# Token mixing with its result transposed, and channel mixing that reads it so

## The reference

```python
theta = x @ w_theta
zr, zi = x * np.cos(theta), x * np.sin(theta)
y = einsum('ts,bsd->btd', w_tok_r, zr) + einsum('ts,bsd->btd', w_tok_i, zi)
u = x + y
m = u + np.maximum(u @ w_ch, 0.0)
gate_pre = sum(conv_w[k] * shifted_by(m, 4 - k) for k in range(5))   # along the tokens
out = (sigmoid(gate_pre) * (m @ w_val)) @ w_out
```

## Time and profile before

| what | value |
|---|---|
| time, median of 3 runs | 741.42 us (741.24 to 741.75) |
| time of the profiled execution | 742.81 us |
| its span (first to last instruction) | 741.0 us |
| PE busy | 688.6 us |
| DVE / ACT / POOL busy | 404.3 / 293.2 / 219.9 us |
| instructions on PE | 3936 matmuls, 3936 weight loads |
| mean granted TensorE clock | 0.97 of full |

### The profile page before, as it was taken

The page is one execution under the profiler, slowest core; times in us unless marked ns, Lnnn a source line. Parts: engine busy times, 40 slices in busy tenths (PEclk is TensorE's granted clock), DMA queues, the critical chain, the costliest instruction groups (busy, mean ns, idle before and its releaser), DMA issues. The chain is left out here.

```text
span 741.0 us, 13752 instructions
## 1 busy us (share of the span) xinstructions
PE 688.6 (93%) x3936; PEld 595.8 (80%) x3936; DVE 404.3 (55%) x973; ACT 293.2 (40%) x752; POOL 219.9 (30%) x267
## 2 busy tenths in 40 slices
PE   4999999999847999999999999987499999999997
PEld 3888888888736888888888888867399999999995
DVE  2666666766517345554564455640936745654770
ACT  3666656666414232231332313313344344435332
POOL 3313223131102221221212212303752463355222
PEclk9999999999969999999999999996889999999999
DMA  5445546464230000600150032064102102200111
GB/s 172 148 139 179 169 149 200 136 189 152 69 119 29 29 15 0 226 19 9 44 182 28 0 140 102 13 206 151 43 1 86 50 35 85 85 24 19 44 43 43
DMA packets 43072, 66.27 MB, mean 89 GB/s; under 512 B 3744, under 2 KB 20384, under 8 KB 42912
## 3 DMA queue, kind: packets, MB, share of 16 engines
q1 hardware_dynamic: 43040, 65.89, 27.4%
HBM read 47.00 MB, written 18.87 MB: 89 GB/s over the span
## 5 line engine op out<-in xcount | busy, mean ns | idle before, releaser
L809 POOL TENSOR_TENSOR z_lo<-z_raw,z_hi 128x512 fp32r<-128x512 f32 x48 | 61.4, 1300 | 213.0 <-ACT z_hi L843 213.0
L245 ACT ACTIVATE probs<-masked,neg_max 128x260 f32<-128x260 f32 (+1 forms) x192 | 92.4, 482 | 69.4 <-DVE neg_max L290 69.2
L972 PE MATMUL acc<-z_hi,w2h 128*128 128x512 f32 x288 | 114.3, 397 | 0.0
L972 PE MATMUL acc<-z_lo,w2h 128*128 128x512 f32 x288 | 112.3, 390 | 0.0
L972 PE MATMUL acc<-z_hi,w2l 128*128 128x512 f32 x288 | 112.3, 390 | 0.0
L290 DVE CUSTOM_DVE_ANT_0 masked<-ps_s,mask 128x260 f32<-128x260 f32 (+1 forms) x192 | 69.0, 403 | 57.7 <-PE ps_s L361 53.7
L1249 DVE SCALAR_TENSOR_TENSOR taps<-m_raw,conv_w,taps 128x384 f32<-128x384 f32 x128 | 76.2, 666 | 0.0
L875 DVE TENSOR_TENSOR xT_lo<-ps_x,xT_hi 128x512 fp32r<-128x512 f32 x24 | 16.6, 690 | 98.3 <-ACT xT_hi L830 98.3
L401 PE MATMUL ps_o<-v_sb,probsT 128*128 128x64 f32 x384 | 66.5, 268 | 0.0
L361 PE MATMUL ps_s<-k_sb,q_sb 64*128 64x260 f32 (+1 forms) x384 | 53.4, 398 | 11.0 <-POOL mask L199 11.0
L972 PEld LDWEIGHTS acc<-z_hi,w2l 128*128 128x128 f32 x288 | 54.1, 188 | 11.7
(11 more groups left out here) (91 smaller groups left out, 1472.9 us busy)
## 6 DMA issues: line engine op xcount, KB each, us to landing
k_sb<-kT SPq DMA_DIRECT2D x16, 396.0 KB, 4.8
q_sb<-qT SPq DMA_DIRECT2D x16, 384.0 KB, 4.3
v_sb<-vP SPq DMA_DIRECT2D x16, 384.0 KB
x_scratch<-x_sb SPq DMA_DIRECT2D x16, 384.0 KB, 3.6
x_nat<-x_scratch SPq DMA_DIRECT2D x24, 256.0 KB, 3.3
x_res<-x_scratch SPq DMA_DIRECT2D x24, 256.0 KB, 4.2
u_scratch<-u_sb SPq DMA_DIRECT2D x24, 256.0 KB, 2.9
u_nat<-u_scratch SPq DMA_DIRECT2D x8, 768.0 KB, 4.6
```

Of the source, the lines that this page charges most:

```text
L245: nc.scalar.activation(probs[e][:, i, lo:hi], masked[2 * t + e][:, lo:hi], ACT.Exp, bias=neg_max[:, s, e, i:i + 1], scale=-1.0, accum_out= ...
L809: nc.gpsimd.tensor_tensor(z_lo[s % ZR][:, part, :], z_raw[:, part, :], z_hi[s % ZR][:, part, :].bitcast(F32), ALU.subtract).then_inc(z_lo_ ...
L972: last = nc.tensor.matmul(acc[t][:], l, r, start=s == 0 and m == 0 and a == 0, stop=s == T - 1 and m == 1 and a == 2)
```

## The change

In block 2, z becomes the stationary operand and the token weights the moving one, so that a bank holds channels by tokens. A result of 512 channels by 768 tokens fills six banks so: bank j < 4 holds channel tile j with tokens 0 to 511 (matmuls of 512 columns), bank 4 holds tokens 512 to 767 of channel tiles 0 and 1, bank 5 those of tiles 2 and 3 (matmuls of 256 columns, two halves in a bank). The residual has to be transposed too: ACT copies `ps_x` once more, to `xT_raw`, SP stores that to a new DRAM tensor `xT_scratch` in rows of 128 tokens, and the residual is loaded from there, bank by bank, once all six tiles of the batch are stored. u is stored transposed (`uT_scratch`).

In block 3, u is loaded as it is needed, so that the 96 transposes, their two banks and ACT's copy to `uT` go. `ps_c` has four banks in place of two. ACT casts `uT` to `uT_hi` (`hi_u`) from SBUF, and does so for chunk n+2 behind the four `hi_m(n+1)`, no longer between those of `hi_g(n)`. In front of the first body it casts chunks 0 and 1, then does `hi_m(0)`. POOL's body is as it was.

```diff
         x_res = [sb(f"x_res{r}", [P, C]) for r in range(RR)]
+        xT_raw = [sb(f"xT_raw{r}", [P, CB, P]) for r in range(XR)]
...
+            def bank_of(scr, b, j):
+
+                if j < CB:
+                    return scr[bass.ds(b, 1), j * P:(j + 1) * P, 0:C].rearrange("o p t -> (o p) t")
+                k = 2 * (j - CB)
+                return scr[bass.ds(b, 1), k * P:(k + 2) * P, C:S].rearrange("o (k p) t -> p (o k) t", p=P)
...
+            def load_res(b, j):
+
+                if j < RR:
+                    for t in range(T):
+                        sp.wait_ge(xT_out[t], 16 * (b + 1))
+                        sp.sem_inc(sp_gate2, 1)
+                sp.wait_ge(u_done, T * (b + 1) + j - RR + 1)
                 sp.sem_inc(sp_gate2, 1)
...
+                sp.dma_start(two_halves(x_res[j % RR], j), bank_of(xT_scr, b, j)).then_inc(res_in[j % RR], 16)
+
+            def store_xT(b, s):
+                sp.wait_ge(xT_raw_done, T * b + s + 1)
+                sp.sem_inc(sp_gate2, 1)
+                sp.dma_start(xT_scr[bass.ds(b, 1), :, s * P:(s + 1) * P].rearrange("o (k p) t -> p (o k) t", p=P),
+                             xT_raw[s % XR][:]).then_inc(xT_out[s], 16)
...
                 act.wait_ge(turned2, n + 1)
+                wait_count(act, xT_out[(s - XR) % T], 16 * (b + 1) if s >= XR else 16 * b)
+                nc.scalar.copy(xT_raw[s % XR][:], ps_x[:]).then_inc(xT_raw_done, 1)
                 wait_count(act, theta_done, n - XR + 1)
                 nc.scalar.copy(xT_hi[s % XR][:], ps_x[:]).then_inc(xT_hi_done, 1)
...
+            def block_of(s, k, bank, cols, first):
+
+                for m in range(2):
+                    at = ((1 - m) * T + s) * S
+                    w = (w2h[:, at + cols.start:at + cols.stop], w2l[:, at + cols.start:at + cols.stop])
+                    z = (z_hi[s % ZR][:, m, k * P:(k + 1) * P], z_lo[s % ZR][:, m, k * P:(k + 1) * P])
+                    for a, (l, r) in enumerate(split_passes(z, w)):
+                        last = nc.tensor.matmul(bank, l, r, start=first and s == 0 and m == 0 and a == 0,
+                                                stop=s == T - 1 and m == 1 and a == 2, skip_group_check=True)
+                return last
...
+                    if j < CB:
+                        last = block_of(s, j, acc[j][:], slice(0, C), True)
+                    else:
+                        for h in range(2):
+                            last = block_of(s, 2 * (j - CB) + h, acc[j][:, h * (S - C):(h + 1) * (S - C)],
+                                            slice(C, S), h == 0)
...
+        ps_c, ps_v, ps_o = banks("ps3_c", CB), banks("ps3_v", 2), banks("ps3_o", 2)
...
-                wait_count(sp, turned, CB * (n - 1))
+                wait_count(sp, m_done, CB * (n - 1))
+                wait_count(sp, uT_lo_done, CB * (n - 1))
                 sp.sem_inc(sp_gate3, 1)
...
+            def hi_u(b, c, k):
                 n = 2 * b + c
...
-                act.wait_ge(turned, CB * n + k + 1)
-                wait_count(act, m_done, CB * (n - 1))
-                nc.scalar.copy(uT[c][:, k, :], ps_t[k % 2][:, 0:L]).then_inc(uT_done, 1)
+                if k == 0:
+                    act.wait_ge(u_in[c], 16 * (b + 1))
+                wait_count(act, mixed, CB * (n - 1))
                 wait_count(act, uT_lo_done, CB * (n - 1))
-                nc.scalar.copy(uT_hi[c][:, k, :], ps_t[k % 2][:, 0:L]).then_inc(uT_hi_done, 1)
+                nc.scalar.copy(uT_hi[c][:, k, :], uT[c][:, k, :]).then_inc(uT_hi_done, 1)
...
                     for k in range(CB):
                         hi_g(b, c, k)
-                        if nxt2:
-                            evac_u(*nxt2, k)
                     if nxt:
                         for k in range(CB):
                             hi_m(*nxt, k)
+                    if nxt2:
+                        for k in range(CB):
+                            hi_u(*nxt2, k)
                     evac_out(b, c)
...
                     for k in range(CB):
                         values(b, c, k)
-                        if nxt2:
-                            turn(*nxt2, k)
```

More of the change, by code:

```diff
@@ L701, in mix_tokens @@
         u_out = [sem(f"u_out{r}") for r in range(RR)]
+        xT_out = [sem(f"xT_out{t}") for t in range(T)]
         w3_in = [sem(f"w3_in{j}") for j in range(4)]
@@ L775, in body @@
                         load_x(b + 1, s - 1)
+                    if s < T - 3:
+                        store_xT(b, s + 3)
+                    elif not last:
+                        store_xT(b + 1, s + 3 - T)
+                    if s == T - 2:
+                        for j in range(RR):
+                            load_res(b, j)
                 if last:
@@ L781, in body @@
                         sp.wait_ge(u_out[r], 16 * T // RR)
[L782 to L785, removed]
+                    sp.dma_start(uT0[:], uT_scr[0, :, 0:S // 2].rearrange("(k p) t -> p k t", p=P)).then_inc(u_in0, 16)
+                for j in range(T):
+                    sp.wait_ge(u_done, T * (b + 1) + j + 1)
                     sp.sem_inc(sp_gate2, 1)
[L787 to L792, removed]
+                    sp.dma_start(bank_of(uT_scr, b, j), two_halves(u_sb[j % RR], j)).then_inc(u_out[j % RR], 16)
+                    if j < T - RR:
+                        load_res(b, j + RR)
                 if not last:
                     load_x(b + 1, T - 1)
+            for t in range(3):
+                store_xT(0, t)
             batches(sp, body)
@@ L959, in theta @@
                 last.then_inc(theta_done, 1)
+            def block_of(s, k, bank, cols, first):
[7 more added lines that the diff above has]
+                return last
             def tokens(b, s):
-                n = T * b + s
-                pe.wait_ge(z_lo_done, 2 * n + 2)
-                for t in range(T):
+                pe.wait_ge(z_lo_done, 2 * (T * b + s) + 2)
+                for j in range(T):
                     if s == 0:
[L966 to L973, removed]
+                        pe.wait_ge(u_done, T * b + j + 1)
+                    if j < CB:
[4 more added lines that the diff above has]
+                                            slice(C, S), h == 0)
                     if s == T - 1:
                         last.then_inc(acc_done, 1)
-                    elif t == T - 1:
+                    elif j == T - 1:
                         last.then_inc(tok_done, 1)
@@ L1020, in mix_channels @@
         w_lo = w3l + [sb("w3_lo2", [P, CB, C], F32R)]
-        u_nat = [u_nat0, sb("u_nat1", [P, UT, C])]
-        uT = [sb(f"uT{r}", [P, CB, L]) for r in range(2)]
+        uT = [uT0, sb("uT1", [P, CB, L])]
         uT_hi = [sb(f"uT_hi{r}", [P, CB, L], F32R) for r in range(2)]
@@ L1034, in mix_channels, with banks @@
         conv_w = sb("conv_w", [P, CB, TAPS])
-        def banks(name):
-            return [ctx.enter_context(nc.psum_tensor(f"{name}{r}", [P, 512], F32)) for r in range(2)]
-        ps_t, ps_c, ps_v, ps_o = banks("ps3_t"), banks("ps3_c"), banks("ps3_v"), banks("ps3_o")
+        def banks(name, count):
+            return [ctx.enter_context(nc.psum_tensor(f"{name}{r}", [P, 512], F32)) for r in range(count)]
+        ps_c, ps_v, ps_o = banks("ps3_c", CB), banks("ps3_v", 2), banks("ps3_o", 2)
         w_in = sem("w3_in2")
@@ L1092, in _, with body @@
             sp.dma_start(conv_w[:], conv).then_inc(conv_in, 16)
-            load_u(1, 0)
-            def body(b, loads):
+            def body(b, last):
                 for c in range(2):
-                    if c < loads:
-                        load_u(b + 1 + c, 1 - c)
+                    if not last:
+                        load_u(b + 1, c)
                     for j in range(UT):
@@ L1105, in body @@
                                      o_sb[j][:]).then_inc(o_out[j], 16)
[L1107 to L1110, removed]
+            batches(sp, body)
             for j in range(UT):
@@ L1210, in _ @@
             for k in range(CB):
-                evac_u(0, 0, k)
+                hi_u(0, 0, k)
             for k in range(CB):
-                evac_u(0, 1, k)
+                hi_u(0, 1, k)
+            for k in range(CB):
                 hi_m(0, 0, k)
@@ L1275, in _ @@
         def _(pe):
[L1276 to L1284, removed]
             def product(m, k, bank, rhs_hi, rhs_lo):
```

52 lines of the change are left out of this document (20 added, 32 removed).

## The result

| kernel | median, us | runs | span of the profiled execution |
|---|---|---|---|
| before | 741.60 | 6 | 741.0 |
| changed | 771.72 | 6 | 769.8 |

The changed kernel is slower by 4.15% (ratio 1.0415, 95% interval 1.0401 to 1.0428). The forecast was 767.9 us within 758 to 784; the loss is 30.1 us where 26.5 were forecast.

What follows compares the result with a forecast made beforehand. The prediction took PE to bound blocks 2 and 3, with DVE nearly as late in block 3. Terms +25.6, -3.9 and +4.8 sum to +26.5 us, on a median of 741.42: 767.9 us, range 758 to 784.

Steps and rivals of the forecast that it cites:

- The wait for m_lo: Block 3, steady part: PE waits 3.7 us before values for POOL's last lo_m, six times.
- The period: Block 3, steady part: outputs 30.3 us apart for six periods, +25.6 us in all.
- the first gated: Block 3, steady part: PE waits 1.7 us for DVE's first gated before values k = 2, six times.
- rival (d): Block 3: PE's pauses drop it to half clock, 1.7 us lost per period, 10 us in all, 778 us; chance 0.17.
- The sixteen instructions: Block 3's steady convolution on DVE: sixteen L1249 take about 14 us instead of 8.55, beside POOL's subtractions.
- The start of block 3: Block 3 up to outputs(0): earlier lo_u, fewer turns, convolution of chunk 0 begins earlier; -3.9 us.
- Block 2: Narrow matmuls +3.4, ACT's extra copy at the begin +1.1, residual loads at the end +0.3: +4.8 us in all.
- the forecast's line through the wider ones: Block 2: 256 column matmuls cost 0.1198 us, from those of 512 and 384 columns; +3.4 us.
- rival (c): Block 2: narrow matmuls cost as much as those of 384 columns, +34.6 instead of +3.4, 799 us; chance 0.08.
- the float32 matmuls as a bound: Block 2: upper bound for 256 column matmuls, 0.26 us each from another type, +84 us.
- (a): Block 3: POOL isn't late, period 24.87 us, in all -6.1, 735.3 us; chance 0.04.
- (b): Block 3: POOL's subtractions take 0.985 us without disturbing the convolution, period 26.2, +1.9, 743.3 us; chance 0.05.

Runs made afterwards that it cites:

- e2: Changed kernel with ACT's hi_u(n+2) put ahead of its hi_m(n+1), POOL's order left as changed: 737.25 us, 0.9942 of the kernel before.
- e1: Changed kernel with POOL's lo_m(n+1) put ahead of its lo_u(n+2), ACT's order left as changed: 759.82 us, ratio 1.0250 to the kernel before.
- e3: Changed kernel with the convolution's accumulators of two of four channel tiles in PSUM, ps_c back at two banks: 758.50 us, ratio 1.0224.
- e6: Changed kernel with 21 unread matmuls behind each outputs(n), n = 0 to 5, ps_c back at two banks: 768.35 us, ratio 1.0350.
- e4: Block 2 of the changed kernel followed by block 3 of the kernel before, reading u in the wrong order: 747.54 us, ratio 1.0075.
- e8: Kernel before, with only POOL's work moved out of block 3's first convolution: 734.37 us, ratio 0.9903.
- e7: Kernel of e2 with POOL's work moved out of block 3's first convolution: 731.88 us, 0.9871 of the kernel before.

## Why the prediction was right, point by point

**The wait for m_lo.** Right in place, cause and number: the last m_lo was forecast at E+11.9 and stood at E+12.05 (E being the first start in the timeline, 0.16 us ahead of the chain's piece that the prediction took in the kernel before). e2 and e1 show the queues' order as the cause, e3 the exclusion.

**The period.** 30.3 was forecast, 30.75 measured (31.1 and 30.4 by turns): 184.5 us for six, +28.3 instead of +25.6. One part of the picture was wrong. The forecast had PE wait 1.7 us for the first gated and held the half clock of rival (d) apart from it. There was no such wait. PE spent those microseconds, and some more, on values k = 0 and 1 at half clock: the first gated was ready at 602.91, E+17.2, and k = 2 began some 0.8 us after it:

```profile
603.69 0.34 PE L1311 MATMUL ps_v<-m_hi,w_hi 128*128 128x384 f32 x1
```

So rival (d) came true, but at 0.77 us per period by e6 and not at 1.7, since, as the prediction had put against it, half of the loss and more fell on time that PE would have waited anyway, the 0.93 us of e6. Without the clock the period would have been 29.98, 0.3 under the forecast. The sixteen instructions took 13.8 to 14.6 us, about the 14 forecast, but when POOL was done DVE had eight left and not ten: three of the first tap, 0.33 us apart, were through before POOL began, and the first gated was there at E+17.2 instead of E+17.8. So the period had two errors, the convolution 0.3 us too long and the clock's 0.77 us at nothing, that cancelled in part; that it came so near is partly luck.

**The start of block 3.** -3.9 forecast; from the block's begin to the first start of outputs(0) it was 52.7 us before (501.50 to 554.22) and is 48.3 now (506.33 to 554.61), -4.4.

**Block 2.** +4.8 forecast. Its length, from the first transpose to the begin of block 3, went from 290.2 to 295.3 us, +5.2, and e4 gives +5.6 (3.9 to 7.2 by its interval). Single traces differ by up to 1 us in it: e8 has the block 2 of before and takes 289.2, e2, e6 and e7 have the changed one and take 295.6 to 296.1. The narrow matmuls stand 0.12 us apart, on the forecast's line through the wider ones:

```profile
369.44 0.28 PE L994 MATMUL acc<-w2h,z_hi 128*128 128x256 f32 x1
369.56 0.28 PE L994 MATMUL acc<-w2l,z_hi 128*128 128x256 f32 x1
369.68 0.28 PE L994 MATMUL acc<-w2h,z_lo 128*128 128x256 f32 x1
369.80 0.40 PE L983 MATMUL ps_th<-w2h,xT_hi 128*128 128x512 f32 x1
```

That settles rival (c), and with it the float32 matmuls as a bound: they were far off for this type. The Trainium skill ("TensorE: Matmul & The Clock Gate", section "Back-to-back issue gap") gives a gap of N/2.4 + 2.5 ns, by estimate 109.2 ns for 256 columns. It gives that for single matmuls, which the prediction didn't say; for a stream of pairs of weight load and matmul, as here, it has another figure, lower at 512 columns. The rows agree with neither: they show 120 ns for 256 columns and 227.8 for 512, and the price of cutting a matmul in two is some 12 ns rather than 2.5. The steps grew by 4.4 us in all (267.2 for 262.8) where 3.4 were forecast, the start of the block by 0.8 for 1.1, its end by nothing that the trace shows: the residuals in rows of 1 KB landed in 3.1 us in the median, faster than before, and DVE waited 1.75 and 0.97 us for the last two, for 1.66 and 0.97 before.

**Rivals (a) and (b)** needed POOL to be in time or out of DVE's way; the timelines show neither. e2 is what (a) would have been, and its 24.87 us period is the one that (a) was priced with.

The sum by terms: +28.3 for 25.6, -4.4 for -3.9, +5.2 for 4.8; with -0.3 us in the attention and +0.1 at the tail, and rounding, it gives the 28.8 us between the spans. The term that was most off is the steady part of block 3, by 2.7 us, and the clock is more than all of it.

## What to carry to other kernels

When a step changes its source (here from a transpose in PSUM to a load in SBUF), look where its instruction now stands in its engine's order, and then at the queue behind it: the engine whose code didn't change paid for the move, and PE behind that one. Moving the three lines of the casts gave back 34 us. Where an elementwise operation on DVE with two SBUF inputs is nearly late, as here, look for POOL's subtractions beside it: an accumulator in PSUM, or another place in the order, takes the conflict away, and in this kernel the same question found some 7 us more that the change had not touched.

## What the runs showed of the hardware that was not expected

TENSOR_SCALAR, one SBUF input only, was held up by POOL too when it wrote to SBUF. In e3 it took 1.16 and 1.19 us so (the second line), where the last chunk's second, with POOL idle, took 0.41. When it wrote to PSUM it was not: in the first chunk the second of a pair ran from 523.66 for 0.61 us inside an m_lo of POOL, and took what it took alone.

```profile
523.13 1.14 DVE L1277 TENSOR_SCALAR ps_x<-m_raw,conv_w 128x384 f32<-128x384 f32 x2
584.03 2.27 DVE L1277 TENSOR_SCALAR taps<-m_raw,conv_w 128x384 f32<-128x384 f32 x2
523.71 1.01 POOL L1162 TENSOR_TENSOR m_lo<-m_raw,m_hi 128x384 fp32r<-128x384 f32 x1 [1.07 <-ACT m_hi L1204]
```

The Trainium skill ("SBUF — State Buffer", section "Who interferes with whom") counts tensor_scalar among those that can enter a mode with two ports and then contend; the trace agrees for the SBUF output.

A busy TensorE can be faster than a resting one: with 126 matmuls added in the pauses the kernel was 3.4 us shorter (e6).

After the four transposes of a step, the first dozen or so matmuls of 512 columns stand 0.23 to 0.235 us apart and the later ones 0.227, in the traces of before, after and e2. The theta matmuls behind the narrow ones begin the same way. The runs don't show why.
